# Attention steps joined in pairs, scores one pair further ahead, another order of loads and fewer operations for the first tables

## The reference, cut to what matters

```python
scores = scale * q @ k.T                       # (2, 8, 768, 768)
keep = (pos_k < n_global) | (0 <= rel < n_local)
dist = n_local where global and not local, else |rel|
scores = where(keep, scores - slope[h] * dist, -1e9)
a = softmax(scores);  x = a @ v                # heads side by side: (2, 768, 512)
h = relu(x @ w_in)                             # 512 -> 1024
gate = sigmoid(conv over seq, 3 taps, of h)
x = h * gate @ w_out                           # 1024 -> 512
h = relu(x @ moe2_w_in); u, v = halves of h    # 512 -> 512 + 512
out = u * (w_spatial @ layernorm(v) + b_spatial) @ moe2_w_out
```

## Time and profile before

| | |
|---|---|
| median of 3 runs | 402.11 us |
| the profiled execution, its own time | 403.13 us |
| its span in the profile | 401.3 us |
| TensorE matmuls busy | 378.8 us (94%), 2270 instructions |
| VectorE busy | 219.9 us (55%) |
| ScalarE busy | 176.9 us (44%) |
| GpSimd busy | 85.0 us (21%) |
| TensorE in the chain that ended last | 86% |
| DMA of `k_sb` in that chain | 5% |

### The profile page before, as it was taken

One profiled execution on the slowest core, in us unless ns is written; L12 is line 12 of the kernel. 1 busy time (PEld: TensorE's weight loads), 2 busy tenths in 40 slices (PEclk: granted clock), 3 DMA queues, 4 the chain that ended last, 5 costly groups with the idle time before them and its releaser, 6 DMA issues.

```text
span 401.3 us, 6215 instructions
## 1 busy us (share of the span) xinstructions
PE 378.8 (94%) x2270; PEld 325.9 (81%) x2270; DVE 219.9 (55%) x619; ACT 176.9 (44%) x447; POOL 85.0 (21%) x171
## 2 busy tenths in 40 slices
PE   6788879899989899999999999999999999999994
PEld 2455657676767678999998899999899999998883
DVE  6576535757574776876996859021485344552000
ACT  3476435555545463885634566021365211112221
POOL 2879854324132232000001102000230000000000
PEclk9899989999989999999999999999999999999998
DMA  7803124322233310142130000000134000001222
GB/s 249 343 3 112 42 113 138 126 73 74 86 100 99 100 41 2 54 122 87 54 105 2 1 2 0 0 2 3 37 105 158 0 0 2 1 2 54 92 94 83
DMA packets 11749, 27.70 MB, mean 69 GB/s; under 512 B 1472, under 2 KB 3520, under 8 KB 11712
## 3 DMA queue, kind: packets, MB, share of 16 engines
q1 hardware_dynamic: 11568, 27.23, 20.0%
q10 hardware_dynamic: 144, 0.00, 0.0%
HBM read 24.08 MB, written 3.15 MB: 68 GB/s over the span
## 4 chain that ended last, share of the span: by engine, by line
PE 86%; DMA 5%; POOL 3%; DVE 3%; issue 1%; SPq 1%; ACT 0%; DVEq 0%; POOLq 0%
PE bank L1431 18%; PE bank L1433 18%; PE bank L1432 18%; PE bank L1402 17%; DMA k_sb<-in_k 5%; PE bank L1381 5%; PE bank L1340 5%; PE bank L1361 4%; PE bank L1408 1%; POOL p_sb L537 1%; DVE p_sb L953 1%; POOL bias L529 1%; DVE pt_sb L970 1%; POOL w_lo L549 1%; SPq L471 1%
## 5 line engine op out<-in xcount | busy, mean ns | idle before, releaser
L1402 PE MATMUL bank<-xT,w_hi 128*128 128x384 f32 x256 | 76.4, 362 | 0.0
L537 POOL TENSOR_SCALAR p_sb<-p_sb,denom 128x256 f32<-128x256 f32 (+1 forms) x96 | 47.3, 506 | 77.2 <-DVE denom L964 77.1
L953 DVE CUSTOM_DVE_ANT_0 p_sb<-bank,bias 128x256 f32<-128x256 f32 (+1 forms) x96 | 33.0, 399 | 49.8 <-PE bank L1340 30.6
L627 ACT ACTIVATE p_sb<-p_sb,row_min 128x256 f32<-128x256 f32 (+1 forms) x96 | 46.3, 485 | 12.4 <-DVE row_min L953 12.3
L1402 PEld LDWEIGHTS bank<-xT,w_hi 128*128 128x128 f32 x256 | 45.7, 191 | 7.3 <-issue 7.1
L635 ACT COPY pt_sb<-bank 128x512 f32<-128x512 f32 (+1 forms) x41 | 22.7, 553 | 58.2 <-PE bank L1361 58.2
L1402 PE MATMUL bank<-xT,w_lo 128*128 128x384 f32 x128 | 46.3, 362 | 0.0
L1431 PE MATMUL bank<-g_hi,w_hi 128*128 128x386 f32 (+1 forms) x128 | 43.3, 338 | 0.0
L1433 PE MATMUL bank<-g_hi,w_lo 128*128 128x386 f32 (+1 forms) x128 | 43.2, 337 | 0.0
L1432 PE MATMUL bank<-g_lo,w_hi 128*128 128x386 f32 (+1 forms) x128 | 43.1, 336 | 0.0
L990 DVE SCALAR_TENSOR_TENSOR c_sb<-h_sb,conv_sb,c_sb 128x382 f32<-128x382 f32 (+1 forms) x64 | 41.7, 652 | 2.3
(11 more groups left out here) (93 smaller groups left out, 744.5 us busy)
## 6 DMA issues: line engine op xcount, KB each, us to landing
stage<-in_weights SPq DMA_DIRECT2D x19, 512.0 KB, 3.3
v_sb<-in_v SPq DMA_DIRECT2D x8, 390.0 KB, 3.2
k_sb<-in_k SPq DMA_DIRECT2D x8, 384.0 KB, 4.2
out_dram<-out_sb SPq DMA_DIRECT2D x12, 256.0 KB, 2.0
q_sb<-in_q SPq DMA_DIRECT2D x13, 192.0 KB, 3.6
v_sb<-in_v SPq DMA_DIRECT2D x5, 260.0 KB, 2.7
k_sb<-in_k SPq DMA_DIRECT2D x5, 256.0 KB, 3.8
v_sb<-in_v SPq DMA_DIRECT2D x1, 780.0 KB, 8.8
```

The lines of the kernel that those rows point to most:

```text
L537: nc.gpsimd.tensor_scalar(probs_h, probs_h, denom[:, u % SLOTS, h:h + 1], 1.0, ALU.mult, ALU.mult).then_inc(scaled, 1)
L627: nc.scalar.activation(p_sb[:, u % SLOTS, h, 0:n], p_sb[:, u % SLOTS, h, 0:n], ACT.Exp, bias=row_min[:, u % SLOTS, h:h + 1], scale=-1.0, a ...
L953: nc.vector.tensor_tensor_reduce(out=p_sb[:, u % SLOTS, h, 0:n], in0=score_bank(u, h)[:, u % 2 * 2 * P:u % 2 * 2 * P + n], in1=bias[:, 2 * ...
L1402: last = nc.tensor.matmul(banks[5 + j % 3][:, 0:C], w, x, start=r == 0, stop=r == F1_GROUP - 1)
```

## The change

TensorE now works two units in one step: `turn_probs(u)`, 5 `f1`, `turn_probs(u+1)`, 3 `f1`, then `weigh(u-2)`, `weigh(u-1)` and `scores(u+6)` in a row, then 8 `f1`. Scores start three pairs ahead (0, 2 and 4 before the loop), ScalarE's `soften` four units ahead instead of three, and `pt_sb` has four slots. `round_x`, `rest_of_x`, `relu_h` and the taps move to steps that fit. On SyncE, queries and keys (`load_queries`) are loaded ahead of the values of a triple two earlier (`load_values`); the second head pair has transfers of its own, the first values and the convolution weights go out on ScalarE's queue, and the chunks 1 to 3 go to buffers that need no waiting (two in a new `stage_late`). Chunk 0 is split by ScalarE and VectorE in two halves of 512 columns around units 6 to 9, chunks 1 to 3 by GpSimd in six pieces of 512 columns at units 13 to 18. The distance table is one piece with another column order; heads 2 to 4 get their tables on GpSimd before any scaling, heads 5 to 7 at units 1, 3 and 5; ScalarE makes most of head 0's table. `WARM` is 10.

```diff
-WARM = 14
+WARM = 10
-EARLY = 3 * P
+AT_T1, AT_LATER, AT_T0 = 0, 2 * P, 4 * P
+PT_SLOTS = 4
-PIECE = 256
+PIECE = 512
-PIECE_FIRST = 6
+PIECE_FIRST = F1_FIRST - 1
+        stage_late = put("stage_late", [P, 2, WCH], F32, "late")
...
+        def round_step(p):
+            return 2 * ((TG * p + TG - 1) // 2 + 1) + 1
+        def relu_step(j):
+            pair, r = divmod(F1_GROUP * (j + 1) - 1, 2 * F1_STEP)
+            return F1_FIRST + 2 * pair + (1 if r < F1_STEP else 2)
...
             sp.dma_start(k0_sb[:, 0, :], k0[0]).then_inc(k_first, 16)
-            sp.dma_start(v0_sb[:, 0, :], v0[0]).then_inc(v_first, 16)
-            sp.dma_start(q0_sb[:, 1:HP, :], ...
-            sp.dma_start(k0_sb[:, 1:HP, :], ...
-            sp.dma_start(v0_sb[:, 1:HP, :], ...
+            sp.dma_start(q0_sb[:, 1, :], q[1]).then_inc(q_second, 16)
+            sp.dma_start(k0_sb[:, 1, :], k0[1]).then_inc(k_second, 16)
+            sp.dma_start(q0_sb[:, 2:HP, :], ...
+            sp.dma_start(k0_sb[:, 2:HP, :], ...
+            sp.dma_start(v0_sb[:, 1, :], v0[1]).then_inc(v_second, 16)
+            sp.dma_start(v0_sb[:, 2:HP, :], ...
             load_chunk(0)
-            load_chunk(1)
-            sp.dma_start(conv_sb[:], conv_w).then_inc(conv_in, 16)
-            load_pair(HP)
-            load_pair(HP + 1)
-            for n in range(2, NW1 + 2):
+            load_queries(HP)
+            load_queries(HP + 1)
+            load_values(HP)
+            load_values(HP + 1)
+            for n in range(1, NW1):
                 load_chunk(n)
-                load_pair(HP + n)
-            for pg in range(HP + NW1 + 2, ALL_TRIPLES):
-                load_pair(pg)
+            load_queries(HP + 2)
+            load_queries(HP + 3)
+            for pg in range(HP + 2, ALL_TRIPLES):
+                if pg + 2 < ALL_TRIPLES:
+                    load_queries(pg + 2)
+                load_values(pg)
+            load_chunk(NW1)
+            load_chunk(NW1 + 1)
...
-            scale_probs(0)
-            pool.wait_ge(tables, TABLE_STEPS)
+            for n in range(2, 5):
+                table(n)
             for u in range(ALL_UNITS):
-                if u >= 1:
-                    scale_probs(u)
-                if u < HP - 1:
-                    table(2 * u + TABLE_HEADS)
-                    table(2 * u + TABLE_HEADS + 1)
-                if PIECE_FIRST <= u < PIECE_FIRST + NW1 * PIECES:
+                scale_probs(u)
+                if u in (1, 3, 5):
+                    table(5 + u // 2)
+                if PIECE_FIRST <= u < PIECE_FIRST + (NW1 - 1) * PIECES:
                     split_piece(u - PIECE_FIRST)
...
-            for u in range(3):
+            act.wait_ge(tables, DIST_STEPS)
+            nc.scalar.activation(bias[:, 0, 0:AT_T0], dist[:, 0:AT_T0], ACT.Copy, scale=slope8(0) * UNIT
+                                 ).then_inc(table_of_0, 1)
+            for u in range(4):
                 soften(u)
             for u in range(STEPS):
                 if u < ALL_UNITS and not turned_on_dve(u):
                     copy_pt(u)
-                if u + 3 < ALL_UNITS:
-                    soften(u + 3)
+                if u + 4 < ALL_UNITS:
+                    soften(u + 4)
+                if u in (6, 8):
+                    round_half(u // 2 - 3)
                 for j in range(F1_GROUPS - KF):
-                    if F1_FIRST + (F1_GROUP * (j + 1) - 1) // F1_STEP == u - 1:
+                    if relu_step(j) == u:
                         relu_h(j)
...
+            link(nc.vector.scalar_tensor_tensor(count_f[:, 0:2], high, 2.0 ** 32, low, ALU.mult, ALU.add))
+            link(nc.vector.scalar_tensor_tensor(dist[:, 0:TW], rel[:], nl, behind[:], ALU.is_ge, ALU.max))
+            dve.wait_ge(nl_scaled, 1)
+            link(nc.vector.tensor_scalar(reach[:], key[:], ng, count_f[:, 6:7], ALU.is_ge, ALU.add))
+            link(nc.vector.tensor_tensor(near, near, reach[:], ALU.min))
...
+            for h in range(2):
+                link(nc.vector.tensor_scalar(bias[:, h, AT_T0:TW], dist[:, AT_T0:TW], slope8(h) * UNIT, None, ALU.mult))
             bias_scores(0)
+            link(nc.vector.tensor_scalar(bias[:, 1, 0:AT_T0], dist[:, 0:AT_T0], slope8(1) * UNIT, None, ALU.mult))
+            dve.wait_ge(table_of_0, 1)
             bias_scores(1)
             invert_sums(0)
-            table_part(1)
+            bias_scores(2)
             invert_sums(1)
-            bias_scores(2)
             bias_scores(3)
...
-            pe.wait_ge(consts, 9)
             scores(0)
             scores(2)
+            scores(4)
+            pe.wait_ge(consts, 9)
             f1_next = 0
-            for u in range(STEPS):
-                for stage_no, n in enumerate((3, 3, 2)):
-                    if stage_no == 0 and u < ALL_UNITS:
-                        turn_probs(u)
-                    if stage_no == 1 and 1 <= u <= ALL_UNITS:
-                        weigh(u - 1)
+            for u in range(0, STEPS, 2):
+                for stage_no, n in enumerate((5, 3, 8)):
+                    if stage_no < 2 and u < ALL_UNITS:
+                        turn_probs(u + stage_no)
                     if stage_no == 2:
-                        if u % 2 == 0 and u + 4 < ALL_UNITS:
-                            scores(u + 4)
+                        if u >= 2:
+                            weigh(u - 2)
+                            weigh(u - 1)
+                        if u + 6 < ALL_UNITS:
+                            scores(u + 6)
                     if u >= F1_FIRST:
                         for _ in range(n):
                             f1(f1_next)
```

More of the change, by code:

```diff
@@ L7 @@
 I32 = mybir.dt.int32
+U32 = mybir.dt.uint32
 ALU = mybir.AluOpType
@@ L263, in build_program @@
         val_in = [sem(f"val_in{slot}") for slot in range(2)]
-        chunk_in = [sem(f"chunk_in{i}") for i in range(2)]
+        chunk_in = [sem(f"chunk_in{i}") for i in range(4)]
         stored = [sem(f"stored{i}") for i in range(2)]
@@ L475, in load_pair, with load_values @@
                     sp.dma_start(k_sb[:, slot, :], k1[pair]).then_inc(k_in[slot], 16)
+            def load_values(pg):
+                g, hp = divmod(pg, HP)
+                b, c = divmod(g, 2)
+                slot, n = pg % 2, pg - 2
+                pair = b * HP + hp
                 if n >= HP:
@@ L528, in table @@
             def table(n):
-                nc.gpsimd.tensor_scalar(bias[:, n, :], dist[:], slope8(n) * UNIT, 1.0, ALU.mult, ALU.mult
+                nc.gpsimd.tensor_scalar(bias[:, n, :], dist[:, 0:TW], slope8(n) * UNIT, 1.0, ALU.mult, ALU.mult
                                         ).then_inc(later_tables, 1)
+            pool.wait_ge(tables, 3)
+            nc.gpsimd.tensor_scalar(count_f[:, 6:7], count_f[:, 1:2], 1.0 / UNIT, 1.0, ALU.mult, ALU.mult
+                                    ).then_inc(nl_scaled, 1)
+            pool.wait_ge(tables, DIST_STEPS)
             def scale_probs(u):
@@ L706, in _ @@
                     copy_pt(u)
-                if u + 3 < ALL_UNITS:
-                    soften(u + 3)
+                if u + 4 < ALL_UNITS:
+                    soften(u + 4)
+                if u in (6, 8):
+                    round_half(u // 2 - 3)
                 for j in range(F1_GROUPS - KF):
-                    if F1_FIRST + (F1_GROUP * (j + 1) - 1) // F1_STEP == u - 1:
+                    if relu_step(j) == u:
                         relu_h(j)
-                if u >= TG and u % TG == 0:
-                    round_x(u // TG - 1)
+                for p in range(ALL_TRIPLES):
+                    if round_step(p) == u:
+                        round_x(p)
             relu_h(F1_GROUPS - KF - 1)
@@ L1083, in _ @@
                     bias_scores(u + 5)
+                for p in range(ALL_TRIPLES):
+                    if round_step(p) + 1 == u:
+                        rest_of_x(p)
+                if u in (7, 9):
+                    rest_of_half((u - 7) // 2)
                 if u == GU + 2:
@@ L1328, in score @@
                     if hp == 1 and tt == 0:
+                        pe.wait_ge(q_second, 16)
+                        pe.wait_ge(k_second, 16)
+                    if hp == 2 and tt == 0:
                         pe.wait_ge(q_rest, 16)
```

124 lines of the change are left out of this document (68 added, 56 removed).

## The result

The changed kernel takes **375.57 us** (median of 4 runs, 374.75 to 375.96) against 402.06 us for the kernel before (4 runs): ratio 0.934, interval 0.932 to 0.936, or 26.5 us less. The forecast was 379.5 with a range of 373 to 388, so it went in the right direction and was 4 us too cautious. The profiled execution took 375.65 us with a span of 373.8; the one before took 403.13 with 401.3.

What follows compares the result with a forecast made beforehand. Bound by idle time and clock dips in TensorE's first 160 us, and by GpSimd in the first stage; 11.5 + 6.5 - 0.5 + 7.3 + 0.5 - 1.8 - 0.8 = 22.7 us, so 380.4 profiled, 379.5 median; range 373 to 388.

Steps and rivals of the forecast that it cites:

- Loads: Second stage: earlier queries and keys remove all five key waits and the clock dips behind them, 11.5 us (8.0 to 11.5).
- Joined steps: Pair steps on TensorE: fewer changes of kind between `f1` and attention blocks save 6.5 us (bounds 0 and 6.5).
- rival that blocks in a row save nothing: TensorE's joined blocks cost as much in a row as apart, through their waits: 6.5 go, 386 us; chance 0.08.
- Second transpose waits for ScalarE's copy: In each pair, the second transpose needs the bank ScalarE must have emptied: 0.5 us lost over 18 pairs (0 to 2).
- First stage: Up to unit 14: early tables and GpSimd left only the scaling bring unit 14 to 34.7 against 42.00, 7.3 us won.
- The limit that it named: First stage after GpSimd: VectorE is the next limit, 2.8 us a pair, 3.4 with its wait and half chunks.
- GpSimd behind it: Pieces at units 13 to 18: unit 15 waits 1.8 us, a possible clock dip costs 0.8, a `scores` already done wins 0.5.
- The last stage: From the start of the last stage to the end, the time must stay what it is, 241 us.
- GpSimd's pieces slowed by VectorE: Units 17 and 18: four operations a unit each 0.3 us longer, 2.4 us, so 382 us; chance 0.10.

## Why the prediction was right, step by step

The terms held in their order, and the loads and the joined steps in their mechanism. One part fell outside its own bounds, though: the joined steps gave 8.2 where the upper bound was 6.5. In the first stage the size came out and the limit named only in part. The result lies 0.6 us above the lower end of the forecast's own range of 375 to 384.

- **Loads, 11.5 predicted.** 11.3 by the run with the loads alone, in the time and in the start of the second layer. The clock was 1.00 once the waits had gone; the lower bound of 8.0 was not needed.
- **Joined steps, 6.5 predicted.** The mechanism was right and the size off: 8.2 by the run that undoes it, 8.9 by its marks. The step assumed that blocks in a row cost what they cost apart less the 0.20 in the `f1` rows. The pair compared above shows 0.43 in the `f1` rows and another 0.14 inside the block. The rival that blocks in a row save nothing is excluded by the same run.
- **Second transpose waits for ScalarE's copy, 0.5 lost.** No such wait is in the list. In a pair the first transpose starts at 110.12, the copy at 110.76 for 0.58, and the second transpose at 111.44, behind its five `f1`: the cover was enough. It is 1.32 us by these rows (the terms in the prediction add up to 1.29, not 1.31), and the copy ended 0.10 ahead of it.
- **First stage, 7.3 won.** 8.4. Unit 2 at 13.41 was forecast at 13.2, unit 14 at 33.56 was forecast at 34.7. The tables give 3.8 to 4.5 of it (with the clock that goes with them), the place of the pieces 4.1; together that is near the whole, though the two runs each undo one part and say nothing of how the parts act on each other. The step had counted the tables without the clock, which was 0.96 over this stage and is now 1.00. Its sum has a slip: 17.5 and four pairs of 3.4 are 31.1, not 31.7, for unit 13, which came at 30.5. The limit that it named holds only in part. From unit 4 (16.81) to unit 14 (33.56) TensorE's listed waits are 0.24 and 0.38 us for GpSimd's scaling and 0.42 for VectorE's copy, 1.04 of 16.75 us. Nearly all the rest is its own work: the pair from 29.96 has 1.02 of transposes, 1.03 of weighing and 1.06 of scores, 3.1 us, a term that the prediction did not set beside VectorE's. So TensorE was the next limit, with VectorE's work close behind it; that VectorE's 3.4 us a pair came near the 3.3 measured (from unit 4 to unit 12, 13.15 us for four) is in part luck.
- **GpSimd behind it, 1.8 and 0.8 lost, 0.5 won.** Too gloomy. Unit 15 waits for 0.81 us and not 1.8 (1.03 with what is unlisted: it comes 2.35 after unit 14, where the plain distance is 1.32), and no clock dip followed. With T = 30.5 for unit 13, unit 14 came at T + 3.1 as forecast, but held up at the end by VectorE's copy (0.42), not by the scaling, which GpSimd began at 32.42. Unit 15 came at T + 5.4 and not T + 6.1. Two things are in that: a unit takes GpSimd 2.87 us (32.42 to 35.29, rows below) and not 3.05, and unit 15's first transposes start when the first of the two heads is scaled, 0.62 us after the scaling began. The 0.5 was not measured by itself.
- **The rest.** The last stage is 222.28 against 222.15 us, unchanged as said. The clock is 1.00 from 0 to 151.5 us.

The sum: 11.3 + 8.2 + 8.4 + 0.5 - 0.8 = 27.6 us, against 27.5 in the span. So close a match is luck, for the 0.5 is the forecast's and unmeasured, and the joined steps are 8.2 by the time and 8.9 by the marks. In medians the gain is 26.5: the profiled execution before stood 1.0 above its median, that of after only 0.1. The forecast of 22.7 was short by 1.7 in the joined steps, 1.1 in the first stage, and 2.3 in losses of 3.1 that came to 0.8. Much of it is one habit: small interferences were counted in full, and gains only where a row showed them.

**GpSimd's pieces slowed by VectorE**, the third rival, is there on a small scale, and so is the reverse. GpSimd's and VectorE's timelines of after, side by side:

```profile
32.42 0.93 POOL L585 TENSOR_SCALAR p_sb<-p_sb,denom 128x256 f32<-128x256 f32 x2
...
34.03 1.28 POOL L597 TENSOR_TENSOR w_lo<-stage,w_hi 128x512 fp32r<-128x512 f32 x1
35.29 0.93 POOL L585 TENSOR_SCALAR p_sb<-p_sb,denom 128x256 f32<-128x256 f32 x2
```

```profile
34.00 0.17 DVE L1012 RECIPROCAL denom<-denom 128x2 f32<-128x2 f32 x1
34.08 1.25 DVE L1010 TENSOR_SCALAR denom<-denom 128x2 f32<-128x2 f32 x1
```

```profile
L1010 DVE TENSOR_SCALAR denom<-denom x48: 146/161/1249, 9.4 to 122.7; 128x2 f32<-128x2 f32 x48
```

The last row is the group of all 48 additions, with the shortest, the median and the longest in ns. The addition of two columns takes 0.16 us in the median. Here it takes 1.25 and ends at 35.33, when GpSimd's subtraction ends at 35.31. The Trainium skill's page "SBUF — State Buffer" (section "Who interferes with whom") says that a GpSimd instruction and a VectorE instruction that takes the ports they share, which a `tensor_scalar` can, exclude each other for a whole instruction. The trace agrees. From unit 18 on, beside VectorE's taps, the rival's own direction shows: a scaling of 1.33 us (at 43.87) and one rounding of 0.91 (at 45.17), where they take 0.93 and 0.62 elsewhere, and the scalings of two units in 2.23 (at 47.43) where they take 1.84 (at 50.43), 1.1 us in all. All six subtractions kept their 1.28 us. That is less than the 2.4 us of the rival, and no wait of TensorE follows it: after 33 us its only listed ones are the 0.42 for VectorE's copy and the 0.81 for the scaling of unit 15.

## What to carry to other kernels

Each block of attention matmuls that stood apart among the `f1` cost 0.26 us here, so such blocks belong together where other engines allow it; but coarser steps need a look-ahead that fits in every engine's loop: with TensorE's scores one pair less ahead and the other loops left as they were, the kernel was 62.6 us slower. Order the transfers on a queue by when each one's slot comes free and when it is wanted, not by what belongs together: that alone was 11.3 us. Side work of a helper engine belongs where TensorE has a stock of work that waits for nobody, and when a step is made faster, look at what was queued beside it for the next wait.

## What was not expected of the hardware

- A wait early in the kernel can cost more than its length: 2.9 us of waits for tables went with 10 us at half the clock, and the kernel lost 4.5 us. With more waits, the clock was 0.62 over 50 us.
- The granted clock can read 1.00 near the start of a profile while matmuls take nearly twice their time (2.08 us for eight, 1.13 in another profile of the same kernel).
- Two `weigh` of eight matmuls in a row take 1.02 us, and 0.59 each apart.
- An addition of 128x2 elements on VectorE lasted 1.25 us beside a subtraction of GpSimd, eight times its median.
